# A fused mLSTM and two feed-forward layers on one core: the causal mask folded into unused rows of the gate product, gate rows copied by DMAs, three gate segments

## The chip, the cores and the metric

The kernel runs on one core of a Trainium2 chip. The metric is the device time of one execution in microseconds (us), for the slowest core, which here is the only one. Three runs of the kernel before took 469.27, 471.08 and 480.05 us (median 471.08). A difference under 2% (9.4 us) counts as no change.

The engines are named as in the profile: PE is TensorE (matmuls), PEld its weight loads, DVE is VectorE, ACT is ScalarE, POOL is GpSimd, SP is SyncE, which here only issues DMAs. SPq is SP's queue.

## What is computed

Three layers, one after the other. The first is a recurrent attention (mLSTM) over 768 steps for 2 x 8 heads of 40 channels; the other two are feed-forward layers over the 1536 tokens.

```python
# first layer, B, H, S, D = 2, 8, 768, 40
for t in range(S):
    m_new = np.maximum(f_gate[:, :, t] + m, i_gate[:, :, t])
    f_stab = np.exp(f_gate[:, :, t] + m - m_new)
    i_stab = np.exp(i_gate[:, :, t] - m_new)
    m = m_new
    C = f_stab[:, :, None, None] * C + i_stab[:, :, None, None] * np.einsum('bhd,bhe->bhde', vt, kt)
    n = f_stab[:, :, None] * n + i_stab[:, :, None] * kt
    h_tilde = np.einsum('bhde,bhe->bhd', C, qt)
    nq = np.einsum('bhd,bhd->bh', n, qt)[:, :, None]
    y[:, :, t] = sigmoid(o_gate[:, :, t]) * h_tilde / np.maximum(np.abs(nq), 1.0)
# second layer: x (1536 x 320), w_in (320 x 2048), w_out (2048 x 320)
h = x @ w_in
g = (a[0] + a[1]*h + a[2]*h**2 + a[3]*h**3) / (1.0 + abs(b[0])*abs(h) + abs(b[1])*h**2 + 1e-06)
x = g @ w_out
# third layer: w_gate, w_val (320 x 1536), w_out (1536 x 320)
xn = x / rms * rms_g;  gate = xn @ w_gate
out = (gate * sigmoid(gate) * (xn @ w_val)) @ w_out
```

## The kernel before

The whole kernel is one program with an instruction list for each engine, written out by hand. Each list runs in the order in which it is written, and semaphores (`wait_ge`, `then_inc`) are all that holds the engines together.

The first layer is cut into chunks of 128 time steps (`L`). One step of its loop (`it`, 0 to 11) handles one chunk `c = it // 2` of one batch `b = it % 2` with its 8 heads. In a chunk the recurrence becomes matrix products. The weight of key position j for query position l in head h is `exp(A[h, l] + B[h, j])` where j is not after l, and 0 otherwise. A is the running sum of the gate steps (`cumA`), and B is the input gate less the running maximum and less that sum (`i_g`). Both come from `gif`, the gates, on 16 partitions (one for each batch and head), by scans and subtractions on DVE and POOL. The kernel before does this in two segments: `SEG[0]` is chunks 0 and 1, `SEG[1]` is chunks 2 to 5. Each value is split in a high part (rounded to fp32r) and a low part (the rest).

One matmul pair makes the exponents of one `it`, `A + B` for 8 heads x 128 queries in PSUM (`log_weights`, L1448):
- the stationary operand is `gB`, 128 rows x 128 key positions: B high in rows 0 to 15, B low in rows 32 to 47, ones in rows 64 to 127;
- the moving operand is `sel`, 128 rows x (16 heads x 128 queries): rows 0 to 63 hold constant zeros and ones that pick a head's row of B, rows 64 to 127 hold A high and A low, laid out by head. These rows are filled anew for every `it`: on ACT by eight ACTIVATEs, one for each head (`spread`, L738), and for it 0, 1 and 5 by one DVE instruction (`spread_whole`, L1104);
- two matmuls in front of it (`causal`, L1433) put -1e30 above the diagonal into the same PSUM banks by an identity matrix.

Then, for each `it`: ACT takes the exponential of the 128 x 1024 exponents (`weights`, L812, tile E). PE makes the scores k.q (`scores`, L1423), and DVE multiplies them with E (`probs`, L1139). PE multiplies that with v (`intra`, L1474), multiplies the carried state with q (`carry`, L1461), and makes the new state (`updates`, L1484) from `wv`, v weighted by E's last column (`weigh`, DVE L1132, two inputs in SBUF). DVE adds the parts (`combine`, L1157 and L1160), makes the denominators (`denominators`, L1180 to L1184) and the state (`state`, L1171 and L1173). POOL decays the state (`decay`, L512), multiplies with the output gate (`gated`, L569, tile yo) and divides (`normalised`, L578 and L581). PE transposes the result for the next layer (`transposes`, L1502), ACT and DVE split it (x_hi L771, x_lo L1196). In between, ACT, POOL and DVE round and split the next layer's weights (L518, L526, L622, L778 to L792, L1191); POOL's last ones stand between its first `denominator` calls (L589), which belong to the second layer's rational function.

On PE, step `it` of the loop does: causal and log_weights of it + 1, carry(it), scores(it + 1), transposes(it - 3), intra(it), updates(it). Matmuls over `warm` (L1388) are filler that computes nothing. Loads are issued by SP in a fixed order; q, k and v have four buffers. The output gate's sigmoid (`output_gates`) needs another table on ACT than the exponential: a table load comes before it and one behind it.

Of the kernel before, what the change touches and what calls it, by code (L numbers as in the profile page):

```python
# [18 lines left out]
P = 128  # L19
B, H, S, D = 2, 8, 768, 40  # L20
BH = B * H
L = P
# [16 lines left out]
SEG = (slice(0, 2 * L), slice(2 * L, S))  # L39
# [3 lines left out]
ON_DVE = 5  # L43
# [10 lines left out]
def build(nc, gates, q_k, kv_n, o_n, a_c, b_c, g_c, w1_main, w1_rest, w1_out, w2_main, w2_rest, w2_out, out):  # L54
    ctx = ExitStack()
    with ctx:
# [89 lines left out]
        mask_f = at("mask_f", [P, P])  # L146
        ends = at("ends", [BH, NC, BH])
# [4 lines left out]
        gB = at("gB", [P, S], F32R)  # L152
# [51 lines left out]
        psD_all = ps[:, 2:4, :].rearrange("p b (h l) -> p (b h) l", **heads)  # L204
        psD1 = [ps[:, 5 + i, :].rearrange("p (h l) -> p h l", **heads) for i in range(2)]
# [82 lines left out]
        low_b_done = sem("low_b_done")  # L288
        ends_ready = sem("ends_ready")
# [73 lines left out]
        def segment(c):  # L363
            return min(c // 2, 1)
# [5 lines left out]
        def _(sp):  # L370
# [27 lines left out]
            sp.dma_start(sig_o[:, 0:FIRST_O, :], o_n[:, 0:FIRST_O, :]).then_inc(o_in[0], 16)  # L398
            load_att(0)
            load_att(1)  # L400
            load_att(2)
# [46 lines left out]
        def _(pool):  # L448
# [9 lines left out]
            own(pool.memset(gA[:, :].bitcast(F32), 0.0))  # L458
# [17 lines left out]

            def input_steps(i):
# [12 lines left out]
            def low_of_b(i):  # L490

                part = SEG[i]
                pool.wait_ge(b_hi, i + 1)
                pool.tensor_tensor(gB[32:32 + BH, part], i_g[:, part], gB[0:BH, part].bitcast(F32), ALU.subtract)\
                    .then_inc(low_b_done, 1)
                pool.wait_ge(low_b_done, i + 1)
# [129 lines left out]
            pool.wait_ge(b_done, 1)  # L626
            pool.tensor_scalar(gB[0:BH, SEG[0]], i_g[:, SEG[0]], 1.0, None, ALU.mult).then_inc(b_hi, 1)
            pool.wait_ge(b_hi, 1)
            ones(0)
            ones(1)  # L630
            for it in range(NT - 1):
                if it == 2:
                    low_of_b(1)
                if it + 2 < NT:
                    ones(it + 2)
                if it == 0:
                    input_steps(1)
# [5 lines left out]
                if it == 1:  # L643
                    input_sums(1)
# [63 lines left out]
        def _(act):  # L708
# [18 lines left out]
            def gate_rows_b(i):  # L727

                act.wait_ge(b_done, i + 1)
                act.activation(gB[0:BH, SEG[i]], i_g[:, SEG[i]], ACT.Copy).then_inc(b_hi, 1)  # L730

            def spread(it):

                c, b = divmod(it, B)
                act.wait_ge(low_a_done, segment(c) + 1)
                act.wait_ge(d_done, it - B + 1)
# [1031 lines left out]
```

## Time and profile before

| | |
|---|---|
| runs | 469.27, 471.08, 480.05 us |
| the profiled execution | 468.82 us |
| its span, first to last instruction | 467.0 us |
| PE busy | 455.5 us (98%) |
| DVE, ACT, POOL busy | 328.5, 289.4, 250.6 us |
| granted TensorE clock | full in all of the span |

The profiled execution's span is 1.8 us shorter than its time. "Busy" is the time in which an engine had an instruction running, waits inside one for a port among it. In the span's 40 equal slices, each digit is the busy share in tenths:

```profile
PE   8999999988999999999999999999999999999997
DVE  7999997998899998999999543484343444534333
ACT  6788887799889999999988648532111222211111
POOL 4476698858898897988989555981000000000000
DMA  8998930230000000000005030000010000100001
```

A slice is 11.7 us. The first layer fills the first six to seven slices, the second the next fifteen, the third the rest. In the chain of waits the profile goes back from the last instruction to what released it. In the timeline, each row has start (us), duration (us), engine, line, operation, output <- inputs, and in brackets the idle time before it with what ended it.

### The profile page before, as it was taken

Reading aid. Unit: us, or ns where it says so; the run is one execution under the profiler, and the core shown is the slowest. Engines: PE = TensorE matmul, PEld = TensorE weight load, DVE = VectorE, ACT = ScalarE, POOL = GpSimd, SP = SyncE. Lnnn points to the kernel's source line nnn. Section 1 sums busy time; section 2 is a strip of 40 time slices with the busy share of each in tenths; the row PEclk is TensorE's granted clock in tenths of the full one; section 3 lists DMA queues with packets and bytes.
Section 4 is the critical chain, followed back from the end, with each engine's and each line's share of the span. In section 5 each row is a group of like instructions: output and inputs, shape, how many; then the busy total and the mean of one; then the engine's idle time right before and its main releaser. Section 6 shows DMA issues by size and latency. Waiting matters only on the chain.

```text
span 467.0 us, 7429 instructions
## 1 busy us (share of the span) xinstructions
PE 455.5 (98%) x2679; PEld 398.8 (85%) x2680; DVE 328.5 (70%) x462; ACT 289.4 (62%) x468; POOL 250.6 (54%) x271
## 2 busy tenths in 40 slices
PE   8999999988999999999999999999999999999997
PEld 4888997866999888998899888888888888888886
DVE  7999997998899998999999543484343444534333
ACT  6788887799889999999988648532111222211111
POOL 4476698858898897988989555981000000000000
PEclk9999999999999999999999999999999999999999
DMA  8998930230000000000005030000010000100001
GB/s 245 332 317 267 268 92 1 91 135 1 0 1 1 1 1 1 0 1 0 2 0 214 2 135 3 0 1 0 1 56 1 0 0 1 44 14 1 1 0 58
DMA packets 8372, 26.78 MB, mean 57 GB/s; under 512 B 1216, under 2 KB 3136, under 8 KB 7824
## 3 DMA queue, kind: packets, MB, share of 16 engines
q1 hardware_dynamic: 8336, 26.30, 17.6%
q8 instruction: 22, 0.36, 0.3%
q14 instruction: 14, 0.11, 0.1%
HBM read 24.33 MB, written 1.97 MB: 56 GB/s over the span
## 4 chain that ended last, share of the span: by engine, by line
PE 82%; DVE 5%; ACT 3%; issue 2%; POOL 1%; DVEq 0%; POOLq 0%; ACTq 0%
PE ps L1620 7%; PE ps L1621 7%; PE ps L1622 7%; PE ps L1550 6%; PE ps L1552 6%; PE ps L1551 6%; PE ps L1568 4%; PE ps L1569 4%; PE ps L1570 4%; PE ps L1528 4%; PE ps L1526 4%; PE ps L1527 4%; PE ps L1624 3%; PE ps L1625 3%; PE ps L1474 2%; PE ps L1529 2%
## 5 line engine op out<-in xcount | busy, mean ns | idle before, releaser
L992 ACT ACTIVATE ab<-ps 128x512 f32<-128x512 f32 x36 | 21.6, 599 | 117.6 <-PE ps L1625 117.6
L1337 DVE TENSOR_TENSOR ab<-ps,ab 128x512 f32<-128x512 f32 x36 | 24.9, 691 | 84.7 <-ACT ab L992 84.7
L589 POOL TENSOR_TENSOR qq<-qq,ab 128x512 f32<-128x512 f32 x48 | 61.2, 1296 | 20.9 <-ACT qq L836 20.8
L595 POOL TENSOR_TENSOR g_lo<-cc,g_hi 128x512 fp32r<-128x512 f32 x48 | 61.9, 1310 | 6.0 <-ACT g_hi L858 6.0
L1550 PE MATMUL ps<-wo_hi,g_hi 128*128 128x320 f32 x192 | 59.9, 312 | 2.1 <-POOL g_lo L595 1.1
L1552 PE MATMUL ps<-wo_hi,g_lo 128*128 128x320 f32 x192 | 59.3, 309 | 0.0
L1551 PE MATMUL ps<-wo_lo,g_hi 128*128 128x320 f32 x192 | 59.3, 309 | 0.0
L1568 PE MATMUL ps<-wo_hi,g_hi 128*128 128x320 f32 x136 | 42.0, 309 | 0.2 <-ACT g_hi L1000 0.2
L1570 PE MATMUL ps<-wo_hi,g_lo 128*128 128x320 f32 x136 | 42.0, 309 | 0.0
L1569 PE MATMUL ps<-wo_lo,g_hi 128*128 128x320 f32 x136 | 42.0, 309 | 0.0
L1550 PEld LDWEIGHTS ps<-wo_hi,g_hi 128*128 128x128 f32 x192 | 36.0, 188 | 5.7 <-issue 2.6
L1526 PE MATMUL ps<-x_hi,w_hi 128*128 128x512 f32 x96 | 38.3, 399 | 1.9 <-DVE cc L1208 1.9
L1203 DVE SCALAR_TENSOR_TENSOR cc<-cc,coef_a,ps 128x512 f32<-128x512 f32 x48 | 35.6, 742 | 3.8 <-ACT cc L828 3.8
L1528 PE MATMUL ps<-x_hi,w_lo 128*128 128x512 f32 x96 | 38.1, 397 | 0.0
L1527 PE MATMUL ps<-x_lo,w_hi 128*128 128x512 f32 x96 | 37.9, 394 | 0.0
L1343 DVE TENSOR_TENSOR cc<-ps,ab 128x512 f32<-128x512 f32 x36 | 24.9, 691 | 17.8 <-PE ps L1625 17.6
L1551 PEld LDWEIGHTS ps<-wo_lo,g_hi 128*128 128x128 f32 x192 | 36.0, 188 | 1.6
L819 ACT ACTIVATE ab<-ps 128x512 f32<-128x512 f32 x48 | 28.6, 596 | 13.7 <-PE ps L1530 12.7
L1208 DVE SCALAR_TENSOR_TENSOR cc<-cc,coef_a,ps 128x512 f32<-128x512 f32 x48 | 35.8, 747 | 1.5
L1552 PEld LDWEIGHTS ps<-wo_hi,g_lo 128*128 128x128 f32 x192 | 36.0, 188 | 0.0
L1213 DVE SCALAR_TENSOR_TENSOR ab<-qq,one_eps,ps 128x1024 f32<-128x1024 f32 x24 | 30.7, 1278 | 6.3 <-ACT ps L852 6.2
L828 ACT ACTIVATE cc<-ps,coef_a 128x512 f32<-128x512 f32 x48 | 32.5, 677 | 0.0
(189 smaller groups left out, 1252.5 us busy)
## 6 DMA issues: line engine op xcount, KB each, us to landing
qk<-q_k_dram SPq DMA_DIRECT2D x12, 448.0 KB, 9.0
wo_raw<-w_out_dram SPq DMA_DIRECT2D x7, 640.0 KB, 7.0
kv<-kv_n_dram SPq DMA_DIRECT2D x10, 372.0 KB, 6.9
w_raw<-w_main_dram SPq DMA_DIRECT2D x4, 512.0 KB, 7.7
out_dram<-y_out SPq DMA_DIRECT2D x12, 160.0 KB, 1.9
w2c_raw<-w_main_dram SPq DMA_DIRECT2D x1, 1536.0 KB, 6.2
sig_o<-o_n_dram SPq DMA_DIRECT2D x1, 1280.0 KB, 7.7
rest_raw<-w_rest_dram SPq DMA_DIRECT2D x2, 512.0 KB, 7.6
```

The costliest lines, as they stand in the source:

```text
L589: pool.tensor_tensor(qq[m % 2][:, h, :], qq[m % 2][:, h, :], ab[m % 2][:, h, :], ALU.mult)\
L595: pool.tensor_tensor(glo(n), cc[n // 2 % CR][:, n % 2, :], ghi(n).bitcast(F32), ALU.subtract)\
L1208: dve.scalar_tensor_tensor(part, part, coef_a[:, 1:2], hp[n], ALU.add, ALU.mult).then_inc(p_h, 1)
L1526: pe.matmul(hp[n], hi, x_hi[:, j, k, :], start=(k == 0), stop=False)
L1527: pe.matmul(hp[n], hi, x_lo[:, j, k, :], start=False, stop=False)
L1528: pe.matmul(hp[n], lo, x_hi[:, j, k, :], start=False, stop=False)
L1550: pe.matmul(acc[t], hi, wo1_hi[:, f, :], start=(f == 0), stop=False)
L1551: pe.matmul(acc[t], hi, wo1_lo[:, f, :], start=False, stop=False)
L1552: mm = pe.matmul(acc[t], lo, wo1_hi[:, f, :], start=False, stop=(f == FT1 - 1))
L1568: pe.matmul(acc[t], hi, wo2_hi[:, f, :], start=(f == 0), stop=False)
L1569: pe.matmul(acc[t], hi, wo2_lo[:, f, :], start=False, stop=False)
L1570: mm = pe.matmul(acc[t], lo, wo2_hi[:, f, :], start=False, stop=(f == FT2 - 1))
```

## The change

1. **Mask.** `causal` stays for it 0 and 1 only. For it 2 to 11 the mask lies in the stationary operand: there is a new one, `gBm`, 128 rows x 2 halves x 640 positions (chunks 1 to 5), one half for queries 0 to 63 and one for 64 to 127. Rows 64 to 127 of it hold the mask, row 64 + q for the q-th query of the half, and `sel`'s rows 64 to 127 hold a fixed one-hot pattern. The two matmuls of `log_weights` now go by halves of the queries (8 heads x 64) in place of halves of the heads, still 512 columns each.
2. **Gate rows.** A high and A low go to `sel`'s rows 16 and 17 (for it 2 and up) by two small DMAs of 8 x 128 values for each it, issued on ACT's queue (`rows`). The rows of `gBm` against them hold ones. The eight ACTIVATEs for each it fall away; they stay once, for it 1 (`spread_second`), and `spread_whole` stays for it 0 only.
3. **Three segments.** `SEG` is chunk 0, chunk 1, chunks 2 to 5. The first two run on DVE before the first exponential is used, with parts of the second on POOL.
4. **Sigmoid.** The first `output_gates` moves from before the first exponential to behind the second one and the four DMAs of `rows`, and SP loads its input two tiles later.
5. New fillers and fewer early ones on PE, and the first gate columns (`gate_columns`) later.

The core of the diff:

```diff
-SEG = (slice(0, 2 * L), slice(2 * L, S))
+SEG = (slice(0, L), slice(L, 2 * L), slice(2 * L, S))
...
+            def masks(chunks):
+                part = slice(chunks.start * L, chunks.stop * L)
+                shape = [P - 64, 2, chunks.stop - chunks.start, P]
+                m = mask_h[64:P, :, :].unsqueeze(2).to_broadcast(shape)
+                pool.tensor_tensor(gBm[64:P, :, part].rearrange("p f (c l) -> p f c l", l=L), m, m, ALU.add).then_inc(masked, 1)
+                pool.wait_ge(masked, 1 + min(chunks.start, 1))
...
-            pool.wait_ge(b_done, 1)
-            pool.tensor_scalar(gB[0:BH, SEG[0]], i_g[:, SEG[0]], 1.0, None, ALU.mult).then_inc(b_hi, 1)
-            pool.wait_ge(b_hi, 1)
             ones(0)
+            input_steps(1)
+            input_sums(1)
+            low_of_a1()
+            high_of_b1()
+            low_of_b(1, 2, 1)
             ones(1)
+            pool.wait_ge(v_ready, 2)
+            masks(slice(1, NC - 1))
...
+                heads, tokens = slice(b * H, (b + 1) * H), slice(c * L, (c + 1) * L)
+                act.dma_start(sel[16:17, heads, :].bitcast(F32), gA[b * H:(b + 1) * H, tokens].bitcast(F32)).then_inc(rows_in[b], 16)
+                act.dma_start(sel[17:18, heads, :].bitcast(F32), gA[32 + b * H:32 + (b + 1) * H, tokens].bitcast(F32)).then_inc(rows_in[b], 16)
...
-            output_gates(0)
             weights(0)
+            gate_rows_a(1)
             for it in range(NT - 1):
...
+                weights(it + 1)
                 if it == 0:
+                    rows(2)
+                    rows(3)
+                    output_gates(0)
+                elif it == 1:
                     columns(0)
-                weights(it + 1)
-                if it == 2:
-                    gate_rows_b(1)
-                if it < NT - B and it + 2 != ON_DVE:
-                    spread(it + 2)
-                if it == 1:
-                    gate_rows_a(1)
+                    gate_rows_a(2)
+                elif it == 2:
+                    gate_rows_b(2)
+                    rows(4)
+                    rows(5)
+                elif it + 3 < NT:
+                    rows(it + 3)
...
+            def one_hot(b):
+
+                dve.wait_ge(consts, 2)
+                dve.wait_ge(d_done, b + 1)
+                dve.tensor_copy(sel[64:P, b * H:(b + 1) * H, :].rearrange("p h (f l) -> p (h f) l", l=Q2),
+                                ident[64:P, 64:P].unsqueeze(1).to_broadcast([P - 64, 2 * H, Q2])).then_inc(onehot, 1)
...
             weigh(0)
             probs(0)
-            gate_maxima(1)
+            chunk_ends(0)
+            one_hot(1)
+            gate_maxima(2)
...
-                if it + 2 == ON_DVE:
-                    spread_whole(ON_DVE)
                 if it == 0:
-                    gate_steps(1)
+                    gate_steps(2)
...
+                if it == 0:
+                    gate_sums(2)
+                    chunk_ends(1)
                 denominators(it)
...
                 if it == 0:
-                    gate_sums(1)
-                    chunk_ends(1)
+                    low_of_a(2)
...
+                pe.wait_ge(rows_in[b], 32 * c)
+                for f in range(2):
+                    mm = pe.matmul(psDh[f], gBm[:, f, (c - 1) * L:c * L], sel[:, b * H:(b + 1) * H, f * Q2:(f + 1) * Q2],
+                                   start=True, stop=True)
```

Where instructions stand now, on DVE, from the first step's `weigh` to its state. Before (the plain m_run is the scan `gate_maxima`, cumA the scan `gate_sums`, den and rden are `denominators`):

```order
L1132 TENSOR_TENSOR wv_71<-kv_69,E_75 128x328
L1139 TENSOR_TENSOR E_75<-ps,E_75 128x1024
L1045 SCALAR_TENSOR_TENSOR m_run<-gif,m_run 16x512
L1132 TENSOR_TENSOR wv_72<-kv_70,E_78 128x328
L1139 TENSOR_TENSOR E_78<-ps,E_78 128x1024
L1054 TENSOR_TENSOR a_step<-gif,m_run 16x512
L1055 TENSOR_TENSOR a_step<-a_step,m_run 16x512
L1157 COPY hU_88<-ps 128x328
L1180 SCALAR_TENSOR_TENSOR den<-hU_88 128x8
```

And in the changed kernel, on DVE over the same work:

```order
L1211 TENSOR_TENSOR wv_71<-kv_69,E_75 128x328
L1218 TENSOR_TENSOR E_75<-ps,E_75 128x1024
L1167 TENSOR_TENSOR ends<-cumA,ident 16x16
L1181 CAST sel<-ident 64x1024
L1118 SCALAR_TENSOR_TENSOR m_run<-gif,m_run 16x512
L1211 TENSOR_TENSOR wv_72<-kv_70,E_78 128x328
L1218 TENSOR_TENSOR E_78<-ps,E_78 128x1024
L1127 TENSOR_TENSOR a_step<-gif,m_run 16x512
L1128 TENSOR_TENSOR a_step<-a_step,m_run 16x512
L1236 COPY hU_88<-ps 128x328
L1133 SCALAR_TENSOR_TENSOR cumA<-reset,a_step 16x512
L1167 TENSOR_TENSOR ends<-cumA,ident 16x64
```

The one-hot copy (CAST) stands before the long scan, and the last sums and chunk ends have moved ahead of the first denominators (another CAST stands ahead of the first `wv`).

On POOL, from the first v's ones (kv) to the first decay's neighbourhood. Before:

```order
L627 TENSOR_SCALAR gB<-gif 16x256
L502 MEMSET kv_69 128x8
L502 MEMSET kv_70 128x8
L502 MEMSET kv_74 128x8
L481 TENSOR_TENSOR gif<-gif,m_run 16x512
L502 MEMSET kv_77 128x8
```

And in the changed kernel, on POOL:

```order
L490 TENSOR_TENSOR gBm<-mask_h 64x2x128
L543 MEMSET kv_69 128x8
L503 TENSOR_TENSOR gif<-gif,m_run 16x128
L509 TENSOR_TENSOR gif<-gif,cumA 16x128
L516 TENSOR_TENSOR gA<-cumA,gA 16x128
L528 TENSOR_SCALAR gBm<-gif 16x2x128
L535 TENSOR_TENSOR gBm<-gif,gBm 16x2x128
L543 MEMSET kv_70 128x8
L490 TENSOR_TENSOR gBm<-mask_h 64x2x512
L543 MEMSET kv_74 128x8
L503 TENSOR_TENSOR gif<-gif,m_run 16x512
L543 MEMSET kv_77 128x8
```

The second segment's gate work, and the mask of four chunks (64x2x512), stand between the ones of the first and of the third v.

On ACT, from the mask's rounding to the fourth step's exponential (E), in the changed kernel; before, the 128x1280 sigmoid and its table load stood ahead of the first E, and 8 ACTIVATEs `sel<-gA,sel` behind each E from the second on:

```order
L877 ACTIVATE E_75<-ps 128x1024
L771 ACTIVATE gA<-cumA 16x128
L877 ACTIVATE E_78<-ps 128x1024
L800 DMA sel<-gA 1x8x128
L801 DMA sel<-gA 1x8x128
L800 DMA sel<-gA 1x8x128
L801 DMA sel<-gA 1x8x128
L827 ACT_TABLE_LOAD
L830 ACTIVATE sig_o<-sig_o 128x1280
L831 ACT_TABLE_LOAD
L880 ACTIVATE E_75<-ps 128x1024
```

Four DMA issues, the sigmoid and both table loads now stand between the second and the third exponential.

## Rows read from the trace of the kernel before

**Rows 1.** Windows: stretch, busy us of each engine (instructions), clock, DMA share, GB/s.

```profile
40.00:50.00 10.00, 10.00 (x98) 9.38 (x97) 9.47 (x20) 8.49 (x20) 6.66 (x12) 1.00 0.72 231
56.16:78.85 22.69, 21.91 (x182) 19.20 (x183) 18.80 (x35) 18.72 (x42) 21.12 (x26) 1.00 0.26 79
79.58:91.14 11.56, 11.56 (x74) 10.22 (x74) 10.54 (x18) 8.78 (x13) 11.08 (x11) 1.00 0.28 92
130.00:270.00 140.00, 139.94 (x783) 126.07 (x782) 125.04 (x141) 125.28 (x167) 121.57 (x108) 1.00 0.05 19
```

**Rows 2.** Chain that ended last, in order of time: start us, us, what.

```profile
41.48 0.50 PE ps L1433 x2
41.98 0.46 PE ps L1448 x2
...
46.57 0.77 PE ps L1484 x8
...
49.15 1.09 PE ps L1423 x16
...
50.72 1.71 PE ps L1474 x16
```

**Rows 3.** Timeline of DVE: a wv alone, and one step's wv and E.

```profile
21.73 0.48 DVE L1132 TENSOR_TENSOR wv<-kv,E 128x328 f32<-128x328 f32 x1
...
49.72 1.38 DVE L1132 TENSOR_TENSOR wv<-kv,E 128x328 f32<-128x328 f32 x1
51.19 1.23 DVE L1139 TENSOR_TENSOR E<-ps,E 128x1024 f32<-128x1024 f32 x1
```

**Rows 4.** Timeline of POOL in that step.

```profile
49.93 0.81 POOL L569 TENSOR_TENSOR yo<-hU,sig_o 128x320 f32<-128x320 f32 x1
```

**Rows 5.** Timeline of POOL at the hand-over to the second layer.

```profile
56.16 1.54 POOL L622 TENSOR_TENSOR wo_lo<-wo_raw,wo_hi 128x640 fp32r<-128x640 f32 x1 [2.66 <-DVE wo_lo L1191]
...
79.58 1.28 POOL L589 TENSOR_TENSOR qq<-qq,ab 128x512 f32<-128x512 f32 x1 [0.73 <-ACT qq L836]
```

**Rows 6.** The chain again, at the second pair of POOL products.

```profile
89.92 1.27 POOL qq L589
```

**Rows 7.** Timeline of DVE, gate work of the start.

```profile
4.38 0.41 DVE L1055 TENSOR_TENSOR a_step<-a_step,m_run 16x255 f32<-16x255 f32 x1
...
8.84 1.22 DVE L1104 TENSOR_TENSOR sel<-gA,sel 64x1024 fp32r<-64x1024 f32 x1
10.63 0.50 DVE L1132 TENSOR_TENSOR wv<-kv,E 128x328 f32<-128x328 f32 x1 [0.57 <-ACT E L812]
...
15.47 1.74 DVE L1054 TENSOR_TENSOR a_step<-gif,m_run 16x512 f32<-16x512 f32 x1
17.25 0.68 DVE L1055 TENSOR_TENSOR a_step<-a_step,m_run 16x512 f32<-16x512 f32 x1
```

**Rows 8.** Timeline of POOL, gate work of the start.

```profile
15.39 1.28 POOL L481 TENSOR_TENSOR gif<-gif,m_run 16x512 f32<-16x512 f32 x1
```

**Rows 9.** Timeline of PE: the scores of it 3 and of it 6.

```profile
24.68 1.16 PE L1423 MATMUL ps<-qk 40*128 40x128 f32 x16
...
43.22 1.16 PE L1423 MATMUL ps<-qk 40*128 40x128 f32 x16
```

**Rows 10.** Timeline of ACT: the fifth exponential, the second sigmoid's first load, x_hi.

```profile
29.52 1.02 ACT L812 ACTIVATE E<-ps 128x1024 f32<-128x1024 f32 x1 [1.51 <-PE ps L1448]
30.56 1.28 ACT L766 ACT_TABLE_LOAD   x1
...
35.51 0.49 ACT L771 ACTIVATE x_hi<-ps 128x384 fp32r<-128x384 f32 x1
```

**Rows 11.** DMA issues: output <- input, queue, count, KB each, us to landing.

```profile
out_dram<-y_out SPq DMA_DIRECT2D x12, 160.0 KB, 1.9
...
gain<-g_c_dram SPq DMA_DIRECT2D x1, 160.0 KB, 6.2
```

**Rows 12.** Timeline of SP's queue: one issue.

```profile
43.90 0.43 SPq L418 DMA_DIRECT2D gain<-g_c_dram  x1
```

More of the change, by code:

```diff
@@ L151, in build @@
         gA = at("gA", [64, S], F32R)
-        gB = at("gB", [P, S], F32R)
+        gB = at("gB", [P, L], F32R)
+        gBm = at("gBm", [P, 2, S - L], F32R, offset=wo1_at + (FT1 - 5) * HD * 4)
         cursor[0] = region
@@ L288, in build @@
         low_b_done = sem("low_b_done")
+        low_a1_done = sem("low_a1_done")
+        low_b0_done = sem("low_b0_done")
+        rows_in = [sem(f"rows_in{b}") for b in range(B)]
+        masked = sem("masked")
+        onehot = sem("onehot")
         ends_ready = sem("ends_ready")
@@ L729, in gate_rows_b, with spread_second, rows @@
                 act.wait_ge(b_done, i + 1)
[L730 to L736, printed above, removed]
-                for h in range(b * H, (b + 1) * H):
-                    last = act.activation(sel[64:P, h, :], gA[:, c * L:(c + 1) * L].bitcast(F32), ACT.Identity,
+                if i == 0:
+                    act.activation(gB[0:BH, :], i_g[:, SEG[0]], ACT.Copy).then_inc(b_hi, 1)
+                else:
+                    shape = [BH, 2, S - 2 * L]
+                    act.activation(gBm[0:BH, :, L:], i_g[:, SEG[i]].unsqueeze(1).to_broadcast(shape), ACT.Copy).then_inc(b_hi, 1)
+            def spread_second():
+                act.wait_ge(low_a_done, 1)
+                for h in range(H, BH):
+                    last = act.activation(sel[64:P, h, :], gA[:, 0:L].bitcast(F32), ACT.Identity,
                                           scale=sel[0:64, h, 0:1].bitcast(F32))
                 last.then_inc(spread_done, 1)
-            act.preload_act_table_set("sigmoid_and_others")
+            def rows(it):
+                c, b = divmod(it, B)
+                act.wait_ge(d_done, it - B + 1)
+                if c == 1:
+                    act.wait_ge(rounded_consts, b + 1)
+                    act.wait_ge(low_a1_done, 1)
+                elif c == 2:
+                    act.wait_ge(low_a_done, 2)
+                heads, tokens = slice(b * H, (b + 1) * H), slice(c * L, (c + 1) * L)
+                act.dma_start(sel[16:17, heads, :].bitcast(F32), gA[b * H:(b + 1) * H, tokens].bitcast(F32)).then_inc(rows_in[b], 16)
+                act.dma_start(sel[17:18, heads, :].bitcast(F32), gA[32 + b * H:32 + (b + 1) * H, tokens].bitcast(F32)).then_inc(rows_in[b], 16)
+            act.preload_act_table_set("natural_log_exp_and_others")
             act.wait_ge(consts, 1)
@@ L1111, in _ @@
             low_of_a(0)
-            spread_whole(0)
             low_of_b()
-            chunk_ends(0)
-            spread_whole(1)
+            spread_first()
+            gate_maxima(1)
+            gate_steps(1)
+            gate_sums(1)
+            one_hot(0)
             def coefficients():
```

135 lines of the change are left out of this document (81 added, 54 removed).

## Prediction

> **What bounds the kernel now.** I read the page first: PE is busy in 98% of the span at the full clock, so a change pays only where it takes work or waits from PE, or from what PE waits for. Then the windows by stage. In the second layer PE is busy 139.94 of 140.00 us [rows 1]: what happens ahead of that stretch moves it as a block, and nothing in it is touched. So the question is by how much the second layer's start moves.
>
> The chain in order of time shows a steady step of the first layer: from one mask pair (L1433, 41.48) to the end of `updates` (46.57 + 0.77 = 47.34), where the next one starts, it is 5.86 us, all of it matmuls: 0.50 the mask's, 0.46 the exponents', 1.09 the scores', 1.71 `intra`'s, 0.77 `updates`', and 1.33 for the rest, `carry` (about 0.85) and the transposes (about 0.48) [rows 2]. DVE is nearly as full, 9.47 of 10 us [rows 1], but not all of that is work. A `wv` takes 0.48 us alone and 1.38 in the steady step: it starts at 49.72, while POOL's `yo` runs to 50.74, and ends 0.36 behind that [rows 3, 4]. Both have two inputs in SBUF, and one waits for the other. The same stands in the gate work: a subtraction of 512 columns takes 0.68 us, and 1.74 where POOL runs its own from 15.39 to 16.67 [rows 7, 8].
>
> The third view is POOL's timeline at the hand-over. From 56.16 POOL is busy 21.12 of 22.69 us in 26 instructions, so only issue gaps are left; then it idles 0.73 us ahead of the second layer's first product at 79.58 [rows 5], and is busy 11.08 of 11.56 us to the end of the second pair at about 91.14 [rows 1]. The chain passes through that pair (89.92) [rows 6]. From 56.16 on POOL has 0.73 us of slack, and PE, which seems the bound there, is ahead only until it needs these products.
>
> **The steady step.** The mask pair goes: 0.50 us off PE in each of it 2 to 11, ten times 5.0 us. PE's step becomes 5.36. Can DVE follow? What it waits for is counted from the end of `carry`: at 49.15 POOL's decay starts, `yo` ends at 50.74, `wv` at 51.10, E at 52.42; PE's `intra` ends at 52.43 [rows 2 to 4]. Both paths start at the same point and neither holds the mask, so I take the step at 5.36. ACT loses eight ACTIVATEs for each step and gains two DMA issues, about 0.43 us each by SP's row [rows 12] (0 if ACT only hands them over): no cost but in the sigmoid's step.
>
> **The start.** Nothing here is shown by the trace as such, so each term has two ends. They are read at the scores of it 3 (24.68 before [rows 9]), behind which the loop runs regularly; up to there DVE is the engine that all wait for.
> - Own work of DVE: two one-hot copies of 64x1024 come, one `spread_whole` of that size goes. The nearest row is 1.22 us [rows 7]; a copy with one input could take about half. So +0.2 to +1.2, and I take 1.2. A third segment adds four small instructions. 256 columns take 0.41 and 512 take 0.68 [rows 7], which leaves a fixed 0.14 each: +0.6.
> - POOL's mask of four chunks has 1024 columns. Two of the 512-column products, 1.28 each [rows 5], less a fixed part make 2.5 us in one instruction with two SBUF inputs. In POOL's list it stands behind the second segment's last part, about 12 us, when DVE comes to `ends`, the one-hot copy and the long scan, which feed `wv` and the second E. By the rows on waiting above, DVE stands still for what is left of it: 0 to 2.5, and I take 2.0, since the one-hot copy may run beside it.
> - `gate_sums` now stands ahead of the first denominators, so POOL's 512-column subtraction (1.28 [rows 8]) starts as they do, and they, the state and PE's `updates` behind it wait: 0 to 1.3, and I take 1.3. The stretch of 1.06 on `a_step` before should then go, as POOL will be done by then: 0 to -1.06, and I take -0.6.
> - The first exponential comes earlier: the first segment is half as long, and POOL clears fewer columns. DVE waited 0.57 for it [rows 7]. 0.6 to 1.4, and I take -1.0.
> - The sigmoid with two table loads (1.28 each [rows 10]; about 3.9 us together) now stands between the second and third exponentials. DVE comes to the third `wv` only at the end of the gate work, later still than before: hidden by the terms above. If DVE were early, it would cost about 1 us.
>
> Sum at the scores of it 3: 1.2 + 0.6 + 2.0 + 1.3 - 0.6 - 1.0 = 3.5 us later, from -1.7 (all low ends) to about +5.
>
> The Trainium skill, SBUF — State Buffer, section "SBUF: two separate sides", says that DVE and GpSimd share one pair of SBUF ports as an exclusive lock, held for the whole instruction, against DVE instructions with two SBUF inputs or in a 2-port mode. The trace agrees with the first (1.38 against 0.48). By its further rule that copies can enter a 2-port mode the one-hot copy would be locked out too, and that term would be 2.5 in place of 2.0; no row shows such a copy.
>
> **From there to it 6** took 43.22 - 24.68 = 18.54 us [rows 9]. It held three mask pairs, the third `spread_whole` on DVE and the second sigmoid. After, PE needs 1.09 (scores), 1.71 (intra) and 0.77 (updates) to the exponents of it 4; the exponential follows about 0.7 later and takes 1.02, two issues 0.86, and from the first table load to the end of x_hi it is 36.00 - 30.56 = 5.44 [rows 10]: 11.6 us behind the scores of it 3. Then x_lo, the transposes, intra, updates, exponents and carry, 0.5 + 0.5 + 1.7 + 0.8 + 0.5 + 0.85 = 4.8, give 16.4. So 2.1 us come back, and the scores of it 6 are 1.4 later. One step more at 5.36 leaves 0.9 at the point where POOL's closed stretch begins, after DVE's `wo_lo` [rows 5].
>
> **The hand-over.** The remaining steps bring PE another 2.0 us, but POOL's work from there on is as long as before, and it can only use up its idle 0.73, say 0.65. So the second layer starts 0.9 - 0.65 = 0.3 us later. Against the profiled execution's own time: 468.82 + 0.3 = 469.1. The three timed runs are 0.5, 2.3 and 11.2 above that execution; I add 0.5 and predict 469.6, which is 1.5 under their median.
>
> **The rivals.**
> 1. *As worked out, within 1.5 us of the profiled time.* 0.50.
> 2. *The start costs nothing.* If the long mask finds DVE in instructions with one SBUF input (the E products read PSUM) and the sums' place costs nothing, the start term falls from 3.5 to about 0. The ACT path of the sigmoid then binds as before, so it is all handed on: 469.1 - 3.5 = 465.6, with the offset 466.1. For it speaks that DVE's order has such instructions between; against it that the mask's 2.5 us are twice as long as any of them. 0.25.
> 3. *Slower: the gate rows land late.* The rows for it 4 are issued behind the fourth exponential and a rounding of 1024 columns (1.02 by E's row), so some 3.6 us behind the exponents of it 3; those of it 4 are due 6.5 behind them (exponents 0.46, carry 0.85, gate columns some 1.6, scores, intra, updates 3.57). It decides where landing takes over 2.9 us. The rows give 1.9 with idle DMA engines and 6.2 behind bulk loads on one queue [rows 11], at a time when the DMA engines are full. With 6.2 it costs 3.3: 472.4, with the offset 472.9. Later rows have two steps of time and are hidden either way. Against it: they are small and have a queue of their own. 0.13.
> 4. *The step doesn't fall.* DVE is busy 9.5 of 10 us, and if its waits for POOL don't shrink, the step stays 5.86 and the change gives nothing back but the spread. That loses 0.5 in each of three steps to it 6 and the next: 469.1 + 1.5 = 470.6, with the offset 471.1. Against it stands the common starting point above. 0.10.
>
> By the Trainium skill, DMA: Bandwidth & Descriptors, sections "Anatomy of one DMA" and "Queues, rings and completion order", a small DMA has a fixed cost of about 2.0 us, and an engine serves its queues in turn. An estimate by that page is 2.0 plus a packet's wait, so rival 3 would cost nothing; 1.9 agrees with the figure, and no row here shows a second queue beside full loads.
>
> The last 0.02 are for what breaks more than one of these.
>
> **The range.** From rival 2 with its offset and some more of the early exponential, 465.4, to rival 3, 473.0: that holds the time 8 times in 10. The likeliest case's own range is 468 to 471. For a change of over 2% (9.4 us; less can't be told from no change here) faster, all ten mask pairs and more than that much again would have to arrive: 0.01. Slower by that needs a wait on the gate rows in every step: 0.03.
>
> **What the changed profile would show.** Step: chain pieces with no mask pair between `updates` and the exponents, 5.36 us from scores to scores for it 6 to 9. Start: the scores of it 3 at about 28 us; a DVE scan or `ends` near 12 us stretched to 2 us or more beside POOL's 64x1024 mask; the first denominator stretched over 1 us. Hand-over: POOL without idle from its first `wo_lo` to its second pair of products, and PE waiting more behind 91 us than before. Gate rows: landing under 2.9 us, and no PE wait on a DMA at the exponents of it 4. I am wrong if the scores of it 3 come by 25 us (then rival 2), if PE waits for the rows (rival 3), or if the second layer starts earlier by more than POOL's start of that stretch plus 0.7, which would mean that POOL doesn't bind there.

## The result: the changed kernel is 8.5% slower

| | before | after |
|---|---|---|
| median of 6 runs each | 471.85 us | 511.34 us (510.99 to 511.72) |
| ratio, 95% interval | | 1.085 [1.083, 1.088] |
| the profiled execution's span | 467.0 us | 509.1 us |
| mean granted TensorE clock in it | 1.000 | 0.902 |
| second layer's first product on POOL | 79.58 | 121.66 |

The prediction was 469.6 us in a range of 465.4 to 473.0; the time is 38 us above its upper end. The last row of the table says where to look: of the 42.1 us that the span grew, 42.08 lie ahead of the second layer. From its first product on both kernels take 387.4 us. In all tables the medians are of every execution, and the ratios compare the quicker kind where a kernel had two kinds of execution (x6 and x8 below reach 501.7 and 494.1 us, and their profiles are of the longer kind).

The page of the changed kernel (span; busy time; three of the rows of 40 slices, now 12.7 us each):

```profile
span 509.1 us, 7371 instructions
...
PE 496.1 (97%) x2660; PEld 437.0 (86%) x2661; DVE 328.1 (64%) x466; ACT 272.4 (54%) x407; POOL 257.4 (51%) x281
...
PE   8799999999979999999999999999999999999997
...
DVE  8934556447988899989999974338443444353343
...
PEclk9655555559999999999999999999999999999999
```

The row PEclk, full in all of the span before, falls in the second slice and stands at 5 tenths to the ninth: 1.2 GHz in place of 2.4. PE's own row shows nothing of it, it stays at 9, and DVE's falls from 9 to between 3 and 6 there: DVE now waits for PE, for 1.92 us ahead of its instruction at 28.33, for one. The clock records of the trace put the stretch at 16.86 to 115.85 us. Windows of it, and of a regular piece of it (columns as in [rows 1]):

```profile
16.86:115.85 98.99, 96.91 (x494) 89.91 (x496) 51.90 (x101) 31.47 (x44) 43.97 (x60) 0.50 0.40 133
...
40.00:50.00 10.00, 10.00 (x54) 9.43 (x54) 4.84 (x9) 6.42 (x5) 4.12 (x6) 0.50 0.45 139
```

PE is busy 96.91 of 98.99 us at half clock. In the 10 us for which [rows 1] had 98 matmul records and DVE at 9.47, there are 54 and 4.84. PE's timeline, from the first fall to the return:

```profile
18.44 1.19 PE L1537 MATMUL ps<-sel,gBm 128*128 128x512 f32 x2 [3.17 <-DMA sel<-gA]
...
35.12 2.08 PE L1504 MATMUL ps<-qk 40*128 40x128 f32 x16
...
44.72 2.08 PE L1504 MATMUL ps<-qk 40*128 40x128 f32 x16
...
53.08 1.83 PE L1551 MATMUL ps<-C,qk 104*128 104x82 f32 x8
54.84 2.08 PE L1504 MATMUL ps<-qk 40*128 40x128 f32 x16
...
112.84 1.20 PE L1537 MATMUL ps<-sel,gBm 128*128 128x512 f32 x2
114.07 0.76 PE L1616 MATMUL ps<-x_hi,w_hi 128*128 128x512 f32 x1
...
115.89 0.39 PE L1617 MATMUL ps<-x_lo,w_hi 128*128 128x512 f32 x1
```

PE waits 3.17 us for the gate rows' DMAs at the exponents of it 2, and the clock falls in that wait. Then a step takes 54.84 - 44.72 = 10.12 us, without a gap, in place of 5.86 [rows 2]. The clock comes back at 115.85, at the first layer's end, where PE has run 3.0 us of 512-column matmuls, one behind the other: the last exponents and the second layer's first products.

The loss by place, scores of after less scores of before: it 3, 35.12 - 24.68 = 10.4; it 6, 64.97 - 43.22 = 21.8; it 10, 105.47 - 66.90 = 38.6; it 11, 119.10 - 77.03 = 42.1.

So three suspects stand in one place: the DMA wait, the thinner PE work in the start, and the mask pair that is gone from each step.

### The profile page after: what moved, and what is told of

It is laid out like the page before. It is cut to its first block, busy times and chain, and to the rows that moved or that the text cites. A ratio compares the mean times of both kernels' runs of the same rounds, so it can differ in the third digit from the quotient of the medians.

```text
span 509.1 us, 7371 instructions
## 1 busy us (share of the span) xinstructions
PE 496.1 (97%) x2660; PEld 437.0 (86%) x2661; DVE 328.1 (64%) x466; ACT 272.4 (54%) x407; POOL 257.4 (51%) x281
## 3 DMA queue, kind: packets, MB, share of 16 engines
HBM read 24.33 MB, written 1.97 MB: 52 GB/s over the span
## 4 chain that ended last, share of the span: by engine, by line
PE 90%; DVE 4%; ACT 3%; issue 1%; DMA 1%; POOL 1%; ACTq 0%; POOLq 0%; DVEq 0%
PE ps L1710 6%; PE ps L1711 6%; PE ps L1712 6%; PE ps L1564 6%; PE ps L1640 5%; PE ps L1642 5%; PE ps L1641 5%; PE ps L1658 4%; PE ps L1660 4%; PE ps L1659 4%; PE ps L1504 4%; PE ps L1616 4%; PE ps L1618 4%; PE ps L1617 4%; PE ps L1714 3%; PE ps L1715 3%
## 5 line engine op out<-in xcount | busy, mean ns | idle before, releaser
L1564 PEld LDWEIGHTS ps<-kv,E 128*128 128x128 f32 x192 | 37.4, 297 | 0.7 <-issue 0.4
L1564 PE MATMUL ps<-kv,E 128*128 128x41 f32 x192 | 37.3, 376 | 0.0
L880 ACT ACTIVATE E<-ps 128x1024 f32<-128x1024 f32 x10 | 10.2, 1024 | 48.9 <-PE ps L1537 48.9
L1424 DVE TENSOR_TENSOR cc<-ps,ab 128x512 f32<-128x512 f32 x36 | 24.9, 692 | 17.8 <-PE ps L1715 17.6
```

The costliest lines, as they stand in the source:

```text
L1564: mm = pe.matmul(psO[:, h, :], E[it % 2][:, h, :], v1[r][:, h, :], start=True, stop=True)
```

## Experiments

All of them, in the order of the argument. "Half clock" is the stretch of the profiled execution in which 1.2 GHz was granted, "second layer" the start of its first product on POOL, both in us.

| run | what it is | median | ratio to before | half clock | second layer |
|---|---|---|---|---|---|
| x1_fill | after, filler in the gap | 508.5 | 1.082 [1.079, 1.086] | 14.6-18.0, 24.8-113.6 | 119.23 |
| x2_gap_before | before, with the gap | 481.6 | 1.025 [1.015, 1.035] | 17.8-31.5 | 88.97 |
| x3_hold_loads | after, rows land early | 508.6 | 1.083 [1.079, 1.086] | 22.6-111.3 | 117.17 |
| x4_dense_later | after, dense filler in it 2 | 511.5 | (one run) | 15.5-32.6, 39.4-114.5 | 120.53 |
| x7_before_nomask | before without the pair | 500.1 | 1.060 [1.052, 1.067] | 26.4-104.9 | 109.75 |
| x12_late_nomask | the same from it 7 on | 476.9 | 1.012 [1.004, 1.019] | 62.0-79.1 | 84.94 |
| x8_pair_back | after, pair back | 480.8 | 1.017 [1.013, 1.022] | 16.3-67.5 | 104.10 |
| x9_pair_start | x3, dense start, pair back | 478.8 | 1.014 [1.010, 1.018] | 30.2-47.3 | 89.52 |
| x5_fill2 | x3, dense start, 2 fillers a step | 478.8 | 1.017 [1.013, 1.022] | 29.8-46.8 | 89.19 |
| x6_fill1 | the same, 1 filler a step | 491.7 | 1.023 [1.017, 1.030] | 30.0-98.3 | 110.56 |
| x10_pool_load | before, 4.3 us more on POOL | 477.7 | 1.011 [1.003, 1.018] | 68.8-79.1 | 84.59 |
| x11_before_fill | before, filler at two gaps | 475.6 | 1.006 [1.002, 1.010] | 42.2-45.6 | 83.23 |

The median of before beside these runs was 469.6 to 471.6 us. Under the 2% of the metric x1, x3 and x7 are slower than before; x2, x5, x6 and x8 are unclear, since their intervals reach over 1.02 and begin under it; x9 to x12 count as no change. Where the ratio doesn't tell, the argument goes by the clock and the second layer's start, read in one profiled execution of each.

### Is it the gap? x1_fill, x2_gap_before, x4_dense_later

x1 fills the wait of after, x2 makes such a wait in before, x4 puts dense filler behind it.

```diff
 # x1_fill (after)
             intra(0)
+            warm_up(15)
             log_weights(2)
 # x2_gap_before (before): four row DMAs into a tile that nobody reads
+                        act.dma_start(junk[j:j + 1, :, :], gA[0:H, L:2 * L].bitcast(F32)).then_inc(junk_in, 16)
...
             intra(0)
+            pe.wait_ge(junk_in, 64)
             log_weights(2)
 # x4_dense_later (after)
                 if it == 2:
-                    warm_up(2, 7, KT * P)
+                    warm_up(14, 7, TB)
```

> The changed kernel with 15 filler matmuls of 512 columns on PE between the first intra and the exponents of it 2, where PE stood idle 3.2 us for the gate rows. The rows land no earlier. Theory (the idle stretch lets the TensorE clock fall, and all of the 42 us follow from it): the granted clock stays full in the whole span, the step is 5.4 us, and the time is 466 to 472. Rival (the clock falls because the matmuls of the first layer without the mask pairs are too light, gap or not): the clock still falls somewhere before 50 us and the time stays above 495.

> The kernel before, with its mask pairs and all else, but four row DMAs into an unused place issued on ACT's queue behind the second exponential, and PE waits for them ahead of the exponents of it 2. Theory (a gap of about 3 us on PE at this place is enough): the clock falls to half at about 17 us and comes back only with the second layer's matmuls; over 505 us. Rival (it needs the lighter steps of the changed kernel as well, since with the mask pair of 512 columns in each step the clock comes back): the clock falls for a few steps at most, under 485 us.

> The changed kernel with its gap, but 14 filler matmuls of 512 columns in it 2, behind the carry, in place of 2 of 384. Theory (at half clock the first layer's own matmuls keep PE busy but never bring the clock back, while a few us of 512-column matmuls in a row do, as at the second layer's start): the clock is full again from about 38 us on, about 6 us of filler paid, 478 to 486 us. Rival (the clock comes back only where the work behind it is dense too): it falls again at once or never rises, over 505 us.

x1 came out 2.8 us under after. Its first fall, at 14.56, stands inside the `intra` ahead of the gap's place, so that one doesn't need the gap either (a wait of 0.93 us for DVE ends 2.3 us before it). The clock came back at 17.97 under the fillers and fell again at 24.80, with PE busy in both places:

```profile
13.31 2.52 PE L1564 MATMUL ps<-kv,E 128*128 128x41 f32 x16
...
23.38 2.37 PE L1564 MATMUL ps<-kv,E 128*128 128x41 f32 x16
```

x2 has a longer gap than after, and loses the clock in it too, but gets it back. x2's PE:

```profile
20.48 1.22 PE L1453 MATMUL ps<-sel,gB 128*128 128x512 f32 x2 [4.67 <-DMA junk<-gA]
...
29.81 1.20 PE L1438 MATMUL ps<-mask,identr 128*128 128x512 f32 x2
30.81 0.93 PE L1453 MATMUL ps<-sel,gB 128*128 128x512 f32 x2
31.58 1.02 PE L1466 MATMUL ps<-C,qk 104*128 104x82 f32 x8
```

The mask pair and the exponents pair stand side by side there, four matmuls of 512 columns, and the `carry` right behind them runs at 2.4 GHz again (1.02 us, 1.83 in after). In x4 the clock rises under 14 fillers at 32.60 and falls at 39.42, at the end of the next `intra`:

```profile
32.22 3.16 PE L1469 MATMUL ps<-warm 128*128 128x512 bf16 x13 [0.22 <-issue]
...
37.62 2.01 PE L1564 MATMUL ps<-kv,E 128*128 128x41 f32 x16
```

So the gap is neither needed for the loss (x1) nor enough for it (x2), and one dense burst doesn't mend it (x4). The gap's own price is small: filling it brought 2.4 us of span at the second layer (121.66 to 119.23).

### Is it the landing? x3_hold_loads

SP holds its bulk loads until the first four gate rows have landed.

```diff
             load_att(2)
+            sp.wait_ge(rows_in[1], 32)
             load_att(3)
```

> The changed kernel, but SP holds back the fourth q/k/v tile and the first weight load until the gate rows of it 3 have landed, so fewer bulk bytes stand in the DMA engines when the rows are issued. Theory (the rows land 5 us late because the engines are still working on the bulk loads issued before): from the end of the issue to landing takes under 3.5 us in place of 5.4, PE waits under 1.5 us, the clock stays full, 465 to 472. Rival (the time of a row DMA is its own, whatever else runs): landing stays above 5 us, the gap and the half clock stay, over 500 us.

```profile
15.12 0.71 PE L1538 MATMUL ps<-sel,gBm 128*128 128x512 f32 x2
...
18.18 1.16 PE L1505 MATMUL ps<-qk 40*128 40x128 f32 x16 [0.97 <-DVE E L1219]
20.01 1.95 PE L1565 MATMUL ps<-kv,E 128*128 128x41 f32 x16 [0.67 <-DVE hU L1237]
23.67 1.65 PE L1575 MATMUL ps<-wv,kv 128*104 128x82 f32 x8 [1.71 <-DVE C L1251]
```

The wait for the DMA is gone (the exponents of it 2 stand right behind `intra`, 15.12 for 18.44). The packets of the four DMAs lie at 12.57 to 15.22, the last of each within 0.75 us of its issue's end; in after they lie at 16.03 to 18.54, though all four had been issued by 14.45. Nothing but the hold differs, so the loads were what held them. But the clock falls all the same, at 22.55, in the waits for DVE that the start now has, and stays at half to 111.29.

### Is it the mask pair? x7_before_nomask, x12_late_nomask

Before, with nothing but the pair taken out, from it 2 on in x7 and from it 7 on in x12 (the mask of those steps is left out of the computation).

```diff
             def causal(it):
+                if it >= 2:    # x12: it >= 7
+                    pe.wait_ge(exp_done, 1 if it == 2 else it)
+                    return
...
-                    mm = pe.matmul(psD1[e] if it == 1 else psD[e], gB[:, c * L:(c + 1) * L], sel[:, h0:h0 + HP, :], start=False, stop=True)
+                    mm = pe.matmul(psD1[e] if it == 1 else psD[e], gB[:, c * L:(c + 1) * L], sel[:, h0:h0 + HP, :], start=(it >= 2), stop=True)
```

> The kernel before with one part of the change alone: the mask pairs of it 2 to 11 are left out (the weights of later positions are then not masked, so this run leaves out part of the computation); nothing else differs, no gate row is copied by a DMA. Theory now (the mask pairs, two 512-column matmuls of full height in each step, are what keeps the TensorE clock at its upper level in the first layer; without them the clock falls while PE is busy all the time): the clock falls to half between 20 and 50 us and comes back with the second layer, over 495 us. Rival (it needs the new start, with its gaps and its DMAs): the clock stays full and the time is 464 to 470.

> The kernel before with the two matmuls of the mask left out for it 7 to 11 (above the diagonal of those steps the exponents are then not masked: this part of the computation is left out); it 2 to 6 keep theirs, so the start is that of the kernel before and PE comes to it 7 in the regular step at the full clock. Three questions. (a) Is the rest of a step quick enough without the pair? The prediction's step at the full clock is 5.36 us from scores to scores in place of 5.86; its fourth rival says that DVE holds it at 5.86. The first step or two behind the exponents of it 7 tell. (b) Theory (the pair keeps the clock up): the granted clock falls to half within a few steps of the exponents of it 7, at about 47 us, with PE busy all the time; the steps at half clock take about 10.1 us, and the second layer's first product on POOL comes late by 4 us for each step at half clock, so some 12 to 20 us for three to five of them: 480 to 490 us. Rival (the pair matters only in the thin stretch of the start, where loads and gate work leave PE little): the clock stays full, and five pairs of 0.50 give 2.5 us back ahead of the second layer. (c) In the rival's case POOL decides what arrives: by the prediction's term at the hand-over at most 0.7 us of the 2.5 do, so 466.3 to 467 us of span; without POOL as a bound 464.5. In the theory's case (c) can't be read from this run.

x7 keeps everything of the old start (eight ACTIVATEs, two segments, the sigmoid's place) and comes to the second layer 30.2 us late. Its PE around the fall at 26.36, and a window behind it:

```profile
25.35 2.74 PE L1477 MATMUL ps<-kv,E 128*128 128x41 f32 x16
```

```profile
30.00:40.00 10.00, 10.00 (x55) 9.43 (x54) 7.69 (x15) 6.42 (x5) 4.24 (x7) 0.50 0.80 225
```

PE waits for nothing from 18.61 to the fall. It drops inside an `intra`, sixteen matmuls of 41 columns. Before has the same busy share in that stretch, 7.75 of 7.75 us, and keeps the full clock. Taking out the pair alone does it. x7's stretch ahead of the fall, and all of it at half clock:

```profile
18.61:26.36 7.75, 7.75 (x71) 7.13 (x72) 7.31 (x15) 5.47 (x15) 6.15 (x7) 1.00 1.03 351
26.36:104.86 78.50, 78.47 (x398) 73.02 (x398) 43.87 (x84) 40.77 (x86) 37.84 (x53) 0.50 0.42 131
```

x12 answers two questions at once. Its PE comes to it 7 in the regular step:

```profile
42.86 1.16 PE L1423 MATMUL ps<-qk 40*128 40x128 f32 x16
...
48.26 1.16 PE L1423 MATMUL ps<-qk 40*128 40x128 f32 x16
...
53.67 1.16 PE L1423 MATMUL ps<-qk 40*128 40x128 f32 x16
...
59.08 1.16 PE L1423 MATMUL ps<-qk 40*128 40x128 f32 x16
61.32 0.52 PE L1505 MATMUL ps<-ident,y 128*128 128x128 f32 x3 [1.08 <-DVE x_lo L1196]
61.68 3.17 PE L1477 MATMUL ps<-kv,E 128*128 128x41 f32 x16
```

Three steps at the full clock take 5.40, 5.41 and 5.41 us, so the work is there to be saved. Then PE waits 1.08 us for DVE, and the clock falls at 62.00. It returns at 79.06, under the second layer's first 512-column matmuls. The kernel's ratio is 1.012, no change by the 2%, although it saved three pairs at the full clock. The fall came later than was expected: the clock held for 15 us without the pair, 13 of them without a wait of PE. Whether it would have fallen without the wait of 1.08 us this run can't say. A DVE row of x12 shows whence the 1.08: the `wv` of a step in which both DVE and POOL round `wo`:

```profile
54.35 0.81 DVE L1191 TENSOR_TENSOR wo_lo<-wo_raw,wo_hi 128x640 fp32r<-128x640 f32 x1
...
55.49 1.74 DVE L1132 TENSOR_TENSOR wv<-kv,E 128x328 f32<-128x328 f32 x1
```

Before has the same `wv` of 1.74 us (at 56.32), and its PE waits only 0.15 us at this place: the pairs had hidden the rest.

### Does PE work in its place bring the clock back? x8_pair_back, x9_pair_start, x5_fill2, x6_fill1

x8 is after with the pair put back into banks that the exponents overwrite. x9, x5 and x6 start from x3, with fillers in place of the DVE waits of the start; x9 has the pair back, x5 two fillers and x6 one filler of 512 columns for each step from it 3 on.

```diff
+                if it > 2:                        # x8, x9
+                    for e in range(2):
+                        pe.matmul(psD[e], identr[:, :], mask[:, :].unsqueeze(1).to_broadcast([P, HP, P]), start=True, stop=True)
+                if it > 2:                        # x5: 2, x6: 1
+                    warm_up(2, 2)
                 for f in range(2):
 # x9, x5, x6: the start
-            warm_up(1, 6)
+            warm_up(4, 6)
...
+                if it == 1:
+                    warm_up(3, 6)
                 intra(it)
+                if it == 1:
+                    warm_up(7, 6)
                 updates(it)
```

> The changed kernel with one part undone: in it 3 to 11 the two mask matmuls stand again ahead of the exponents (their result is overwritten). Gate rows by DMAs, segments, sigmoid and the new start stay. Theory (the mask pairs' load on PE holds the clock; the gap for the gate rows alone costs some steps at half clock): the clock falls at about 17 us in the wait for the rows and is back at 30 to 50 us, 476 to 488 us. Rival (the gap decides and the pairs are indifferent): it stays at half to the second layer, over 500 us.

> As before with the mask pairs back, and loads held back for the gate rows and fillers in the start's three waits. Theory: with the start filled and the pairs back the clock stays full in nearly all of the span, and the scores of it 3 stand about 3 us later than in the kernel before, steps of 5.86 us: 470 to 476 us, which is what all of the change but the lighter PE step is worth. Rival (zero fillers as in the run with two fillers, where the clock fell at 29.8 us, and the mask pair weigh the same): it falls between 25 and 50 us again, 476 to 482 us.

> The changed kernel with loads held back until the gate rows have landed, fillers in the three DVE waits of its start, and two 512-column filler matmuls where each mask pair of it 3 to 11 stood. Theory: the fillers do for the clock what the mask pairs did; full clock in the whole span, steps of about 5.8 us, and a time of 467 to 474, which is what the rest of the change (gate rows by DMAs, segments, sigmoid) is worth. Rival (the fillers, whose data are zeros, do not count for the clock, or the new stationary operand is at fault): the clock falls again, over 495 us.

> The same with one filler matmul in each step in place of two. Theory: if half of what the mask pairs did is enough, the clock stays full and steps take about 5.6 us, 1 to 2 us less than with two; if the pair's amount is near the limit, the clock falls in some steps and comes back or stays down, over 475 us. I hold the second for a little likelier.

x8 takes back 30.6 of the 39.5 us with the pair alone; gap and late landing are still in it. x5 takes back 29.8 of x3's 508.6 with work that computes nothing. So it is not the mask as such but PE's load. x5 changes the start and the steps at once, and no run has the dense start alone; that the filler in the steps counts is shown by x6, which has half of it, lies between and scatters from 480.6 to 501.7 us. With the dense start the clock holds through the scores of it 3 and falls behind them, at about 30 us; with pair or fillers it returns 17.1 us later. x5:

```profile
27.77 1.16 PE L1505 MATMUL ps<-qk 40*128 40x128 f32 x16
28.86 2.84 PE L1567 MATMUL ps<-kv,E 128*128 128x41 f32 x16
```

This is the nearest reading of the prediction's start term at the full clock: 27.77 - 24.68 = 3.1 us (x5 holds the loads, and has fillers on PE ahead of these scores). One execution of x9 had a mean clock of 0.996 and a span of 470.9. Executions of before with the same mean clock had 468.3 to 468.5: the changed start with the pair kept costs about 2.5 us even where the clock nearly stays.

### POOL ahead of the second layer, and a steadier before: x10_pool_load, x11_before_fill

```diff
 # x10_pool_load (before): 4.34 us on POOL in it 7
                     split_rest1(1)
+                    for _ in range(28):
+                        own(pool.memset(eps[:, :], 1e-6))
 # x11_before_fill (before)
+                if it == 1:
+                    warm_up(3, 7, KT * P)
                 intra(it)
                 updates(it)
+                if it == 4:
+                    pe.wait_ge(state_done, 5)
+                    warm_up(4)
```

> The kernel before with 28 one-column memsets on POOL, one after the other, added in it 7, some 3.5 to 5 us of POOL in its closed stretch ahead of the second layer's first products; nothing else differs. Theory of the prediction (POOL binds the hand-over, with 0.73 us of slack): the first products' start moves by the added time less about 0.7, the second layer moves with it, 2.5 to 4.5 us more than the kernel before beside it. Rival (POOL has hidden slack, since later waits on PE take it up): under 1.5 us more.

> The kernel before with fillers only: 3 of 384 columns ahead of the second intra, where PE waits 0.5 us, and 4 of 512 columns behind the updates of it 4, where PE waits 1.0 us for DVE. Theory (the kernel before stands near the point where the clock is lost, and its slower runs, with a mean clock of 0.98 to 0.99, lose it for some us): all runs at mean clock 1.00 and 468 to 470 us, median 1 to 3 us under that of the kernel before. Rival (the slower runs have another cause): the same spread as before, 468 to 480.

In x10 POOL's stretch begins 0.61 us earlier than before (55.55) and its last `wo_lo` ends 3.76 later (82.61 for 78.85): the 4.34 us go through it whole. But the later y also made PE wait 2.28 us, the clock fell for 10.2 us, and POOL then waited 1.97 us for the second layer's first product. So it shows that POOL's stretch is closed, and not what slack is behind it; that part is inconclusive.

x11 asked whether before itself can be made steadier (its executions reach 482.0 us, at a mean clock of 0.969). It can't in this way: 475.6 us, and the added wait on the state, 1.96 us, has a fall of the clock of its own. No version ran faster than before.

## Why the prediction was wrong

**The step that failed: "the mask pair goes: 0.50 us off PE in each of it 2 to 11 ... PE's step becomes 5.36".** The sum rests on [rows 1] and [rows 2], read at the full clock, and no term or rival asked whether the clock stays full when PE's work in a step changes. It doesn't. x7 takes away the pair alone and gets 1.060; x8 gives it back to after and gets 1.017. With the pair gone, one pair of 512 columns stood in a step beside matmuls of 41, 82 and 128 columns, and this work did not hold the clock, with PE busy in all 7.75 us ahead of x7's fall and in 78.47 of the 78.50 us at half clock. The row PEclk was read as a constant of the machine, and it was a result of the work on PE.

The Trainium skill, TensorE: Matmul & The Clock Gate, Part 1 ("The HAM clock gate") ties half clock to an idle PE and full clock to a busy one. Here the profile's busy share doesn't tell the two apart: at half clock PE was busy 96.91 of 98.99 us, and x7's clock fell in the midst of work. The measurement decides.

**The step of 5.36 us at the full clock** was right: 5.40, 5.41, 5.41 in x12. Rival 4 (DVE holds it at 5.86) is out for plain steps. Where DVE also rounds `wo`, x12 shows it late by 1.08 us.

**The start term** was 3.5 us, and 3.1 was measured (in x5, with its fillers). Its parts, in the trace of after, on DVE and POOL; those from 16.86 on lie behind the fall of TensorE's clock. DVE:

```profile
9.37 0.69 DVE L1181 CAST sel<-ident 64x1024 fp32r<-64x1024 f32 x1
10.10 0.64 DVE L1211 TENSOR_TENSOR wv<-kv,E 128x328 f32<-128x328 f32 x1
...
12.15 1.18 DVE L1181 CAST sel<-ident 64x1024 fp32r<-64x1024 f32 x1
...
14.67 2.02 DVE L1211 TENSOR_TENSOR wv<-kv,E 128x328 f32<-128x328 f32 x1
...
17.92 0.67 DVE L1127 TENSOR_TENSOR a_step<-gif,m_run 16x512 f32<-16x512 f32 x1
...
21.13 1.23 DVE L1259 SCALAR_TENSOR_TENSOR den<-hU 128x8 f32<-128x8 f32 x1
```

POOL at the same times:

```profile
12.06 0.72 POOL L535 TENSOR_TENSOR gBm<-gif,gBm 16x256 fp32r<-16x256 f32 x1
...
13.46 2.86 POOL L490 TENSOR_TENSOR gBm<-mask_h 64x1024 fp32r<-64x1024 f32 x1
...
21.04 1.29 POOL L509 TENSOR_TENSOR gif<-gif,cumA 16x512 f32<-16x512 f32 x1 [3.03 <-DVE cumA L1133]
```

- One-hot copies: 0.69 where nothing held the first one, not 1.22. The own work was too high by about half a microsecond for each of the two.
- The first exponential: the first `wv` starts at 10.10 without a wait, 0.53 earlier than in [rows 7], although more work of DVE stands ahead of it. The direction of the -1.0 is right; its size can't be read apart.
- The long mask: 2.86 us (2.5 expected), from 13.46, not 12. Its victim is `wv`, 2.02 for 0.5: 1.5 lost. The second copy lost 0.5 beside POOL's L535. Together 2.0, as in the sum, though on other instructions. The copy has one input and was held up: that is the further rule of the Trainium skill, SBUF — State Buffer, section "SBUF: two separate sides", for which no row of before spoke.
- `gate_sums` ahead of the denominators: den 1.23 beside POOL's 1.29, against 0.17 later on: 1.06 of the 1.3.
- The stretch on `a_step`: 0.67 for 1.74, all 1.07 gone where -0.6 was taken.

The nearness of 3.5 to 3.1 is in part luck. The own work was 1.0 too high, the sums 0.2 and the stretch on `a_step` 0.5, which would leave 1.7 to 1.8; what made up the rest of 3.1 (less gain at the first exponential, or x5's fillers) was not measured apart. The low end of the own work comes to 0 by the prediction's own numbers, not +0.2.

**ACT's issues** cost 0.63 us each, the first 1.22, not 0.43:

```profile
11.16 1.22 ACTq L800 DMA_DIRECT2D sel<-gA  x1
12.41 0.63 ACTq L801 DMA_DIRECT2D sel<-gA  x1
```

**Rival 3, late gate rows**, had the right mechanism at the wrong place and size. It was placed at it 4; the rows of it 2, issued while the DMA engines were full, were the late ones (3.17 us of PE). Those of it 4 had time at half clock. With 472.9 as its price it doesn't account for the result: without the wait (x3) the kernel takes 508.6. The prediction's estimate beside it, 2.0 us and a packet's wait, doesn't hold for the rows of it 2: the first issue ended at 12.38 and its first packet moved at 16.03. (The section of the Trainium skill that it names gives the 2.0 us for DMAs that GpSimd issues; these were issued by ACT.)

**The hand-over.** I gave POOL 0.73 us of slack, of which 0.65 could be used up. Where the clock was full through that stretch the idle ahead of the first product is 0.72 or 0.73 again, in x2, x5, x8, x9 and x11, though they come to it between 3.6 and 24.5 us later. x5's:

```profile
89.19 2.52 POOL L631 TENSOR_TENSOR qq<-qq,ab 128x512 f32<-128x512 f32 x2 [0.73 <-ACT qq L905]
```

A slack would vary with who is late. It looks like a latency inside the chain that POOL itself feeds, and then the term is 0, not -0.65; that reading is argued, and no run tested it. In after PE at half clock was last there, and the term played no part.

**The account.** At the full clock, 467.3 us of span would have been my sum. The 99 us at half clock could cost at most 49.5, were all of it PE's; that gives 516.8. Measured are 509.1. Waits on other engines in that stretch that don't double may explain it, and PE in POOL's place as the last at the hand-over; the 7.7 were not taken apart. Taking out the pair alone (x7) makes 30.2 of the 42.1 us at the second layer's start; in after the clock also falls 9.5 us earlier, and the other 11.9 were not taken apart either.

**What stays open.** Which feature of PE's work decides is not settled: matmul width, total load and the share of 40-row operands all changed together when the pair went. The spread of x6, and before's occasional runs above 475 us at mean clocks of 0.969 to 0.988, suggest that before itself stands near the edge. And x9 and x5 lose the clock for 17 us at about 30 us although their start is dense; why there was not followed up.

## What to carry to other kernels

Treat the granted clock as an output of the schedule: where a change takes matmuls off PE, the forecast needs a rival in which the stretch that gets lighter runs at 1.2 GHz, priced from steps at that clock (here 10.12 us for one of 5.40), even when PE is 98% busy. Before trusting such a saving, take out the work alone (as x7 did) and look at the row of the clock, and not only at the busy share. Small DMAs that feed the critical engine should be issued where the bulk loads leave the DMA engines room, as x3 did for the gate rows.

## What the runs showed that I had not expected

- A PE that is busy all the time lost the full clock (x7 at 26.36, x1 at 24.80, x4 at 39.42 us) and then ran for up to 89 us at 1.2 GHz (x1), until the second layer's 512-column matmuls.
- Matmuls that compute nothing, two in each step and some in the start, took the changed kernel from 508.6 (x3) to 478.8 us (x5).
- Four DMAs of 4 KB issued on ACT's queue from 11.16 to 14.45 us moved at 16.03 to 18.54 us beside full loads, and within 0.75 us of each issue's end with SP's loads held.
- A one-input copy on DVE went from 0.69 to 1.18 us beside a POOL product of 0.72 us.
